# Two token tiles of the first MLP that are computed alone: the tile of 384 tokens is put ahead of the tile of 512

## The chip, the cores and the metric

The kernel runs on one core of one Trainium2 chip. The metric is the device time of one execution in microseconds (us), the median over several executions. PE is TensorE (PEld its weight loads), DVE is VectorE, ACT is ScalarE, POOL is GpSimd, SP is the engine whose queue issues most DMAs.

## The reference

Three stages follow one another, all in float32: attention over channels, a gated MLP and a second MLP.

```python
# q, k, v: (1, 6016, 256)
qn = q / (norm(q, axis=1) + 1e-6);  kn = k / (norm(k, axis=1) + 1e-6)
a = softmax(kn^T @ qn / tau)               # 256 x 256
x = v @ a                                  # 6016 x 256
g = x @ w_gate;  x = (silu(g) * (x @ w_val)) @ w_out       # d_ff = 1536
h = x @ w_in;    out = (h * clip(h + 3, 0, 6) / 6) @ w_out2  # d_ff = 2048
```

## The kernel before

The attention matrix is folded into the weights of the first MLP, so the first MLP reads v directly. Float32 products are made of parts: each operand is split into a high part (a rounded copy, fp32r) and a low part (what is left), and one product is three passes on PE: high x high, low x high, high x low (`PASSES`). A 128 x 128 block of weights is loaded for each pass.

The 6016 tokens are 11 tiles of 512 (`BANK`) and one of 384 (`REST`). Ten tiles of 512 go in five pairs, in which seven products stand for eight; the remaining two tiles go alone and first. Before the change tile 0 has 512 tokens and tile 1 has 384. The order of each engine's work is written out by hand, and semaphores tie the engines together:

- PE, `first_alone(i)` (tile i, 12 blocks j of 128 hidden channels, c = 12 i + j): `up(i, j)` is 12 matmuls (gate, then value), which may start when `prod_full` says that DVE has multiplied block c - 2, since the hidden values have two pairs of PSUM banks. From j = 3 on, `down` of block j - 3 follows each `up`: 6 matmuls, of which the first four wait for the high part (`prod_high`) and the last two for the low part (`prod_ready`) of that block. In tile 0 the last two blocks are done by `finish` (12 matmuls, one half of the output after the other, so that the first half already needs the low part of block 11). In tile 1 the last four `down`s are moved into the first two frames of the pairs. All matmuls of a tile are as wide as it has tokens.
- ACT: silu of the gate (L900); then in tile 0 the high part of tile 1's v (L904, behind blocks 5 and 6); in tile 1 casts of the first pair's operands.
- DVE, per block: the multiplication (L1243, one input in PSUM), the cast that makes the high part (L1233, SBUF to SBUF), the subtraction that makes the low part (L1151, two SBUF inputs). In tile 0 it also transposes tile 1's v (L1203, 2 instructions, behind blocks 4 and 5) and makes its low part (L1151 on `vT_odd`, behind blocks 7 and 8). In tile 1 it transposes v of the first pair (behind blocks 1 and 3).
- POOL meanwhile builds the weights of the pairs from the folded ones: `join_up` (L668, 12 instructions), `sum_up` (L675 four subtractions or additions, L689 four casts, L692 four subtractions, for each of three groups of blocks). Its group n = 1 stops ahead of the casts until tile 0's products are all split (`prod_ready`), then it goes on; later it prepares the first pair's operands (L707, L713).
- SP: loads v tile by tile into one buffer (`v_in`) and stores the two lone results (`y_alone`, L535).

These lines set the widths and what PE waits for:

```python
V_LAST_TURNED, V_LAST_CAST = (4, 5), (5, 6)
...
pe.wait_ge(prod_full, c - 1)
...
if n == 1:
    pool.wait_ge(prod_ready, 2 + J1)
```

Of the kernel before, what the change touches and what calls it, by code (L numbers as in the profile page):

```python
# [21 lines left out]
BANK = 512  # L22
# [4 lines left out]
def attention_mlp_mlp_kernel(nc, q, k, v, tau, w_gate, w_val, w_out, w_in2, w_out2, out):  # L27
# [8 lines left out]
    KC = C // P  # L36
    J1, J2 = F1 // P, F2 // P
    PAIRS = N // (2 * BANK)

    REST = N - (2 * PAIRS + 1) * BANK  # L40
# [15 lines left out]


    def tokens_at(n):
        return n * BANK if n < 2 else REST + (n - 1) * BANK

    def tokens_of(n):
        return REST if n == 1 else BANK


    def tile_of(pair, side):
        if pair < PAIRS:
            return 2 + 2 * pair + side
        return 2 + 2 * (pair - PAIRS - (pair > NARROWER)) + side
# [50 lines left out]
    with ctx:  # L119
        def sb(name, shape, dt=fp32, stack=ctx):  # L120
            return stack.enter_context(nc.sbuf_tensor(name, shape, dt))

        def sem(name):
            return ctx.enter_context(nc.semaphore(name))
# [17 lines left out]
        with ExitStack() as attention:  # L142
# [8 lines left out]
            vT_even = sb("vT_even", [P, 2, KC, BANK], fp32r, attention)  # L151
# [5 lines left out]
            with ExitStack() as early:  # L157
                vT_odd_raw = sb("vT_odd_raw", [P, 2, KC, BANK], fp32, early)
            vT_odd = sb("vT_odd", [P, 2, KC, BANK], fp32r, attention)
# [10 lines left out]
        with ExitStack() as first:  # L170
            up_w = sb("up_w", [P, J1, 7, 2, P], fp32r, first)
            down_w = sb("down_w", [P, J1, 2, C], fp32r, first)
# [23 lines left out]
        psum = ctx.enter_context(nc.psum_tensor("psum", [P, 8, BANK], fp32))  # L196
        HID = [psum[:, b, :] for b in range(4)]
        SUMS_OUT = [psum[:, 4 + b, :] for b in range(4)]
# [18 lines left out]
        NOTHING, ANYTHING = nc.const_aps.tensor(0.0, [P, P], fp32), nc.const_aps.tensor(1.0, [P, BANK], fp32)  # L217
        FOLD = [psum[:, 4 + r, :] for r in range(4)]
        SQ = [psum[:, 4 + 2 * h:6 + 2 * h, :].rearrange("p b c -> p (b c)") for h in range(2)]
        V_FIRST = [psum[:, c, :] for c in range(KC)]  # L220

        first_loaded = sem("first_loaded")
        first_squared = sem("first_squared")
# [44 lines left out]
        vT_high = sem("vT_high")  # L268
        vT_ready = sem("vT_ready")
# [45 lines left out]
        full = {x: sem(f"full_{x}") for x in ("L", "R", "1L", "2R", "2L", "1R")}  # L315
# [36 lines left out]
        def by_blocks(bank):  # L352
            return bank.rearrange("p (j c) -> p j c", c=P)
# [50 lines left out]
        V_TURNED = (4, 5)  # L404
# [59 lines left out]
        def pieces_of(pair, side):  # L464
            half, full, rest = (n // SQUARE for n in (HALF, BANK, REST))
            if pair != NARROWER:
                return ((tile_of(pair, side), 0, 0, full),)
            return ((0, half, 0, full - half), (1, 0, full - half, rest)) if side else ((0, 0, 0, half),)


        def stores_before(pair):
# [333 lines left out]
        def _(act):  # L805
# [52 lines left out]

            def vT_evict(c):
                act.wait_ge(v_read, c + 1)  # L860
                nc.scalar.copy(vT_even[:, 0, c, :], V_FIRST[c]).then_inc(vT_high, 1)

            def exponent(h):
                act.wait_ge(max_ready, h + 1)
# [13 lines left out]
            for r, (h, i) in enumerate(GROUPS_OF_FOLD):  # L878
                if r == TURNED_AT:
                    expT_evict(1)  # L880
                g, n = UP_BLOCKS[i]
# [9 lines left out]
            def cast_x(pair, k):  # L891
                act.wait_ge(x_summed, 4 * pair + {3: 2, 4: 3, 5: 4}.get(k, 1))
                nc.scalar.copy(XS[pair % 2][:, k, 0, 0:pair_width(pair)], raw_x(pair, k)).then_inc(x_high, 1)  # L893

            def first_alone(i):
                for j in range(J1):
                    c = i * J1 + j
                    act.wait_ge(gate_ready, c + 1)
                    act.wait_ge(prod_ready, c + 1)
                    nc.scalar.activation(act_out[:, j % 2, 0:tokens_of(i)], HID[2 * j % 4][:, 0:tokens_of(i)], ACT.Silu).then_inc(act_ready, 1)  # L900
                    if i == 0 and j in V_LAST_CAST:
                        b = V_LAST_CAST.index(j)
                        act.wait_ge(v_read, KC + b + 1)
                        nc.scalar.copy(vT_odd[:, 0, b, 0:REST], vT_odd_raw[:, 1, b, 0:REST]).then_inc(vT_high, 1)  # L904
                    if i == 1 and j >= J1 - 7:
                        cast_x(0, j - (J1 - 7))
                if i == 0:
                    keep_y_alone(i)

            def keep_y_alone(i):  # L910
                for c in range(KC):
                    act.wait_ge(y_summed, KC * i + c + 1)
                    if i > 0:
                        act.wait_ge(y_alone_stored, 32)
                    nc.scalar.copy(y_alone[:, c, 0:tokens_of(i)], SUMS_OUT[2 * i + c][:, 0:tokens_of(i)]).then_inc(y_alone_kept, 1)
# [165 lines left out]
        def _(dve):  # L1081
# [31 lines left out]
            half = 2 * C  # L1113
# [36 lines left out]
            def low(dst, full, high):  # L1150
                return nc.vector.tensor_tensor(dst, full, high.bitcast(fp32), ALU.subtract)  # L1151
# [48 lines left out]
            def turn_v(n, c, turned, tokens=BANK):  # L1200
                if c == 0:
                    dve.wait_ge(v_loaded, (n + 1) * (16 * GROUPS))
                nc.vector.transpose(turned.rearrange("p (m t) -> p m t", t=SQUARE),  # L1203
                                    v_in[:, c:tokens // SQUARE * KC:KC, :]).then_inc(v_read, 1)

            def vT_evict(c):
                dve.wait_ge(vT_high, c + 1)
                low(vT_even[:, 1, c, :], V_FIRST[c], vT_even[:, 0, c, :]).then_inc(vT_ready, 1)

            for r, (h, i) in enumerate(GROUPS_OF_FOLD):  # L1210
                if r == TURNED_AT:
                    expT_low(1)
                g, n = UP_BLOCKS[i]
                high, lo = (folded_up(g, h, part, n) for part in range(2))
                dve.wait_ge(fold_high, r + 1)
                nc.vector.scalar_tensor_tensor(lo, by_blocks(FOLD[r % 4]), row_rec[:, h:h + 1], high.bitcast(fp32),
                                               ALU.mult, ALU.subtract).then_inc(fold_ready, 1)
                if r in V_TURNED:
                    turn_v(0, V_TURNED.index(r), V_FIRST[V_TURNED.index(r)])
                if r in TURNED:  # L1220
                    vT_evict(TURNED.index(r))

# [14 lines left out]
            def first_alone(i):  # L1237
                for j in range(J1):
                    c = i * J1 + j
                    a = act_out[:, j % 2, 0:tokens_of(i)]  # L1240
                    dve.wait_ge(act_ready, c + 1)
                    dve.wait_ge(val_ready, c + 1)
                    nc.vector.tensor_tensor(a, HID[(2 * j + 1) % 4][:, 0:tokens_of(i)], a, ALU.mult).then_inc(prod_full, 1)  # L1243
                    split(c)
                    if i == 0 and j in V_LAST_TURNED:
                        b = V_LAST_TURNED.index(j)
                        turn_v(1, b, vT_odd_raw[:, 1, b, 0:REST], REST)
                    if i == 0 and j - 2 in V_LAST_CAST:
                        b = V_LAST_CAST.index(j - 2)
                        dve.wait_ge(vT_high, KC + b + 1)  # L1250
                        low(vT_odd[:, 1, b, 0:REST], vT_odd_raw[:, 1, b, 0:REST],
                            vT_odd[:, 0, b, 0:REST]).then_inc(vT_ready, 1)
                    if i == 1 and j in (1, 3):
                        turn_x(0, j // 2)

# [120 lines left out]
            for i in range(2):  # L1376
                b = LAST_BLOCKS - 2 + i
# [4 lines left out]
        def _(pe):  # L1382
# [105 lines left out]
            for r, (h, i) in enumerate(GROUPS_OF_FOLD):  # L1488
                if r == TURNED_AT:
                    turn_exp(1)  # L1490
                g, n = UP_BLOCKS[i]
# [29 lines left out]
            def down(c, n, banks, w, j, last=False):  # L1521
                pe.wait_ge(prod_high, c + 1)
                for part, m in PASSES:
                    if m == 1:
                        pe.wait_ge(prod_ready, c + 3)
                    for h in range(KC):
                        end = mm(banks[h][:, 0:n], w[:, j, part, h * P:(h + 1) * P], prod[:, c % 4, m, 0:n],  # L1527
                                 start=j == 0 and (part, m) == PASSES[0], stop=last and (part, m) == PASSES[-1])
                        if last and (part, m) == PASSES[-1]:
                            end.then_inc(y_summed, 1)  # L1530
                if not last:
                    end.then_inc(prod_used, 1)
# [89 lines left out]
            def downs_of(f, half):  # L1622
                if f < 2:

                    j = J1 - 4 + 2 * f + half
                    down(J1 + j, REST, SUMS_OUT[2:4], down_w, j, last=j == J1 - 1)
                elif f < SECOND:
                    down_first(f - 2, half)
                elif f == SECOND:
                    for side in range(2):  # L1630
                        down_first(SECOND - 2 + half, side)
                else:
                    for x in ORDER2[2 * half:2 * half + 2]:
                        if (f, x) != (FRAMES - 1, ORDER2[-1]):
                            down_second(f - 1, x)
# [90 lines left out]
```

## Time and profile before

| | before |
|---|---|
| median of 3 runs | 1086.69 us (1086.4 to 1087.62) |
| the profiled execution's own time | 1086.27 us |
| its span, first to last instruction | 1084.5 us |
| PE busy | 1080.3 us |
| DVE, ACT, POOL busy | 780.2, 667.3, 327.7 us |
| tile 0 on PE | 61.18 to 110.14 us |
| tile 1 on PE, up to the first frame | 110.14 to 143.45 us |

A row of the timeline gives the start and the length of an instruction or of a merged run of them, its engine and line, the operation, the tile it writes and those it reads, the shapes, and the count; in brackets stands the idle time before it and what ended it. Matmuls overlap: the step from one start to the next is what one costs, the length also holds its way through the array.

### The profile page before, as it was taken

What the parts mean: (1) busy time and instruction counts of PE and PEld (TensorE: products, weight loads), DVE (VectorE), ACT (ScalarE), POOL (GpSimd) and SP (SyncE); (2) the same over time, 40 slices, a digit from 0 to 9 for tenths busy, and PEclk for the clock granted to TensorE, in tenths of its full rate; (3) what the DMA queues carried; (4) which work ended last, traced back from release to release, by engine and by line L of the source; (5) the groups of instructions that cost most, each with busy time, mean ns of one, the idle gap of its engine ahead of it and who ended that gap; (6) DMA issues with size and microseconds to landing.
All of it is one profiled execution on the core that took longest, in us unless ns stands there. A gap on an engine that the chain in (4) does not pass through costs nothing.

```text
span 1084.5 us, 14748 instructions
## 1 busy us (share of the span) xinstructions
PE 1080.3 (100%) x5052; PEld 915.3 (84%) x5052; DVE 780.2 (72%) x1146; ACT 667.3 (62%) x1169; POOL 327.7 (30%) x247
## 2 busy tenths in 40 slices
PE   9999999999999999999999999999999999999998
PEld 7888998888888888888888888998888888888998
DVE  6788779666666766766678776776776776776766
ACT  8731245665665565566577776676666666666655
POOL 7998545200310220223088431220210210210000
PEclk9999999999999999999999999999999999999999
DMA  9711112002102100101122201111011111110111
GB/s 381 249 34 20 40 34 40 1 1 59 20 1 59 21 1 20 40 1 39 59 59 72 79 1 32 25 24 40 18 18 39 20 20 40 20 20 1 21 20 40
DMA packets 111082, 46.83 MB, mean 43 GB/s; under 512 B 91552, under 2 KB 101024, under 8 KB 111008
## 3 DMA queue, kind: packets, MB, share of 16 engines
q1 hardware_dynamic: 110432, 44.71, 15.0%
q10 hardware_dynamic: 576, 1.18, 0.3%
q8 instruction: 41, 0.67, 0.3%
q14 instruction: 33, 0.27, 0.1%
HBM read 33.55 MB, written 12.32 MB: 42 GB/s over the span
## 4 chain that ended last, share of the span: by engine, by line
PE 99%; DMA 0%; DVE 0%; DVEq 0%; issue 0%
PE psum L1573 47%; PE psum L1595 35%; PE psum L1517 5%; PE psum L1582 4%; PE psum L1527 2%; PE psum L1395 2%; PE psum L1499 2%; PE psum L1427 1%; PE psum L1408 0%; DMA qk_first<-in_k 0%; PE psum L1541 0%; PE psum L1461 0%; PE psum L1474 0%; PE psum L1483 0%; DVE out_sb L1379 0%; PE psum L1693 0%
## 5 line engine op out<-in xcount | busy, mean ns | idle before, releaser
L1595 PE MATMUL psum<-prod,down_w 128*128 128x512 f32 (+1 forms) x1680 | 408.4, 386 | 0.0
L1595 PEld LDWEIGHTS psum<-prod,down_w 128*128 128x128 f32 x1680 | 315.3, 188 | 61.1 <-DVE y_right L1293 0.2
L1573 PE MATMUL psum<-x_even,up_w 128*128 128x512 f32 (+1 forms) x1260 | 302.8, 386 | 0.0
L1573 PEld LDWEIGHTS psum<-x_even,up_w 128*128 128x128 f32 x1260 | 235.4, 188 | 44.5 <-ACT slots L945 0.3
L1573 PE MATMUL psum<-x_odd,up_w 128*128 128x512 f32 x1008 | 245.3, 389 | 0.0
L1573 PEld LDWEIGHTS psum<-x_odd,up_w 128*128 128x128 f32 x1008 | 189.1, 188 | 39.6 <-DVE more_slots L1318 0.4
L1273 DVE TENSOR_TENSOR slots<-psum,slots 128x512 f32<-128x512 f32 (+1 forms) x108 | 74.1, 686 | 122.9 <-ACT slots L953 96.6
L1322 DVE SCALAR_TENSOR_TENSOR prod<-slots,prod 128x512 fp32r<-128x512 f32 (+1 forms) x144 | 100.7, 700 | 32.8 <-ACT prod L996 28.3
L1318 DVE SCALAR_TENSOR_TENSOR slots<-slots 128x512 f32<-128x512 f32 (+1 forms) x120 | 84.2, 701 | 38.0 <-ACT slots L1006 38.0
L996 ACT ACTIVATE prod<-slots 128x512 fp32r<-128x512 f32 (+1 forms) x144 | 90.0, 625 | 28.2 <-DVE slots L1318 28.2
L713 POOL TENSOR_TENSOR x_even<-x_even_raw,x_even 128x512 fp32r<-128x512 f32 (+1 forms) x42 | 54.0, 1295 | 159.5 <-ACT x_even L893 159.5
L1006 ACT ACTIVATE slots<-slots 128x512 f32<-128x512 f32 (+1 forms) x120 | 75.1, 626 | 34.7 <-DVE slots L1273 31.4
L1151 DVE TENSOR_TENSOR prod<-slots,prod 128x512 fp32r<-128x512 f32 x120 | 95.7, 798 | 0.0
L921 ACT CAST prod<-slots 128x512 fp32r<-128x512 f32 x120 | 74.6, 622 | 19.6 <-DVE slots L1278 11.7
L707 POOL TENSOR_TENSOR x_even_raw<-x_even_raw 128x512 f32<-128x512 f32 (+1 forms) x24 | 34.5, 1451 | 167.6 <-DVE x_even_raw L1203 90.2
L1269 DVE TENSOR_TENSOR slots<-psum,slots 128x512 f32<-128x512 f32 (+1 forms) x108 | 73.6, 682 | 8.5 <-PE psum L1573 8.5
L1264 DVE TENSOR_TENSOR slots<-psum,slots 128x512 f32<-128x512 f32 (+1 forms) x84 | 57.3, 682 | 30.4 <-PE psum L1573 30.1
L713 POOL TENSOR_TENSOR x_odd<-x_odd_raw,x_odd 128x512 fp32r<-128x512 f32 x28 | 35.9, 1292 | 121.2 <-ACT x_odd L893 121.2
L707 POOL TENSOR_TENSOR x_odd_raw<-x_odd_raw 128x512 f32<-128x512 f32 x20 | 29.4, 1481 | 122.2 <-PE psum L1573 66.6
L959 ACT ACTIVATE slots<-slots 128x512 f32<-128x512 f32 x60 | 38.1, 635 | 43.5 <-DVE slots L1273 43.5
L937 ACT COPY slots<-psum 128x512 f32<-128x512 f32 x60 | 35.3, 589 | 40.0 <-PE psum L1573 40.0
L1006 ACT ACTIVATE more_slots<-psum 128x512 f32<-128x512 f32 (+1 forms) x48 | 28.3, 589 | 50.7 <-PE psum L1573 50.5
(151 smaller groups left out, 1309.6 us busy)
## 6 DMA issues: line engine op xcount, KB each, us to landing
out<-out_sb SPq DMA_DIRECT2D x38, 128.0 KB, 2.6
v_in<-in_v SPq DMA_DIRECT2D x36, 128.0 KB, 3.2
qk<-in_q SPq DMA_DIRECT2D x8, 512.0 KB, 9.2
qk<-in_k SPq DMA_DIRECT2D x7, 512.0 KB, 10.5
x_odd_raw<-y_rows SPq DMA_DIRECT2D x12, 256.0 KB, 3.3
y_rows<-act_out SPq DMA_DIRECT2D x10, 256.0 KB, 2.1
y_rows<-y_right SPq DMA_DIRECT2D x10, 256.0 KB, 3.0
down_raw<-in_moe_w_out SPq DMA_DIRECT2D x4, 512.0 KB, 3.8
```

Source lines behind the costliest of these rows:

```text
L707: nc.gpsimd.tensor_tensor(raw_x(pair, k), raw_x(pair, a), raw_x(pair, b), ALU.subtract).then_inc(x_summed, 1)
L713: nc.gpsimd.tensor_tensor(low, raw_x(pair, k), high.bitcast(fp32), ALU.subtract).then_inc(x_ready, 1)
L921: nc.scalar.copy(buffer_of(f, x)[:, 0, :], gated_left if x == "L" else kept6(f)).then_inc(high_of[x], 1)
L996: nc.scalar.activation(buffer_of(f, x)[:, 0, :], clipped(x, f), ACT.Copy, scale=1.0 / 6.0).then_inc(high_of[x], 1)
L1006: nc.scalar.activation(clipped(x, f), src, ACT.Relu, bias=3.0).then_inc(relu_of[x], 1)
L1151: return nc.vector.tensor_tensor(dst, full, high.bitcast(fp32), ALU.subtract)
L1269: nc.vector.tensor_tensor(kept1(f), left_sums(f), kept1(f), ALU.add).then_inc(row1_left, 1)
L1273: nc.vector.tensor_tensor(kept7(f), right_sums(f), kept7(f), ALU.add).then_inc(row2_right, 1)
L1318: nc.vector.scalar_tensor_tensor(clipped(x, f), clipped(x, f), 6.0, hidden, ALU.min, ALU.mult).then_inc(full[x], 1)
L1322: nc.vector.scalar_tensor_tensor(buffer_of(f, x)[:, 1, :], clipped(x, f), 1.0 / 6.0, buffer_of(f, x)[:, 0, :].bitcast(fp32), ALU.mult, ALU ...
L1573: end = mm(bank, w[:, u, k, part, :], XS[pair % 2][:, k, m, 0:pair_width(pair)], start=start and (part, m) == PASSES[0], stop=stop and (pa ...
L1595: end = mm(sums_out(pair_of(f), side, h), w[:, j, part, h * P:(h + 1) * P], buffer_of(f, x)[:, m, :], start=start and (part, m) == PASSES[ ...
```

## The change

`tokens_of` gives 384 to tile 0 and 512 to tile 1, and `tokens_at` shifts with it; the views of tile 0 are narrowed and those of tile 1 widened. Each engine issues the same instructions in the same order. The number of matmuls at each width stays the same.

```diff
     def tokens_at(n):
-        return n * BANK if n < 2 else REST + (n - 1) * BANK
+        return 0 if n == 0 else REST + (n - 1) * BANK
 
     def tokens_of(n):
-        return REST if n == 1 else BANK
+        return REST if n == 0 else BANK
...
-        V_FIRST = [psum[:, c, :] for c in range(KC)]
+        V_FIRST = [psum[:, c, 0:REST] for c in range(KC)]
...
             if pair != NARROWER:
                 return ((tile_of(pair, side), 0, 0, full),)
-            return ((0, half, 0, full - half), (1, 0, full - half, rest)) if side else ((0, 0, 0, half),)
+            return ((1, half - rest, 0, half),) if side else ((0, 0, 0, rest), (1, 0, rest, half - rest))
...
-                        nc.scalar.copy(vT_odd[:, 0, b, 0:REST], vT_odd_raw[:, 1, b, 0:REST]).then_inc(vT_high, 1)
+                        nc.scalar.copy(vT_odd[:, 0, b, :], vT_odd_raw[:, 1, b, :]).then_inc(vT_high, 1)
...
-                        turn_v(1, b, vT_odd_raw[:, 1, b, 0:REST], REST)
+                        turn_v(1, b, vT_odd_raw[:, 1, b, :])
...
-                        low(vT_odd[:, 1, b, 0:REST], vT_odd_raw[:, 1, b, 0:REST],
-                            vT_odd[:, 0, b, 0:REST]).then_inc(vT_ready, 1)
+                        low(vT_odd[:, 1, b, :], vT_odd_raw[:, 1, b, :],
+                            vT_odd[:, 0, b, :]).then_inc(vT_ready, 1)
...
-                    down(J1 + j, REST, SUMS_OUT[2:4], down_w, j, last=j == J1 - 1)
+                    down(J1 + j, BANK, SUMS_OUT[2:4], down_w, j, last=j == J1 - 1)
```

On DVE, from the second transposition of tile 1's v in tile 0 to the second subtraction for tile 1's v, the kernel before has these instructions (L1243, L1233, L1151 on `prod` are one block's multiplication, cast and low part):

```order
 L1203 STREAM_TRANSPOSE vT_odd_raw<-v_in 128x384
 L1243 TENSOR_TENSOR act_out<-psum,act_out 128x512
 L1233 CAST prod<-act_out 128x512
 L1151 TENSOR_TENSOR prod<-act_out,prod 128x512
 L1243 TENSOR_TENSOR act_out<-psum,act_out 128x512
 L1233 CAST prod<-act_out 128x512
 L1151 TENSOR_TENSOR prod<-act_out,prod 128x512
 L1151 TENSOR_TENSOR vT_odd<-vT_odd_raw,vT_odd 128x384
```

The changed kernel has in that place:

```order
 L1203 STREAM_TRANSPOSE vT_odd_raw<-v_in 128x512
 L1243 TENSOR_TENSOR act_out<-psum,act_out 128x384
 L1233 CAST prod<-act_out 128x384
 L1151 TENSOR_TENSOR prod<-act_out,prod 128x384
 L1243 TENSOR_TENSOR act_out<-psum,act_out 128x384
 L1233 CAST prod<-act_out 128x384
 L1151 TENSOR_TENSOR prod<-act_out,prod 128x384
 L1151 TENSOR_TENSOR vT_odd<-vT_odd_raw,vT_odd 128x512
```

The instructions and their order are the same; those of tile 0 became narrower and those for tile 1's v wider. POOL's list is the same in both kernels. On SP the loads of v and the two stores of `y_alone` change their sizes, each in its place:

```order
-L501 DMA v_in<-in_v 32x32x32 x4
+L501 DMA v_in<-in_v 32x24x32 x4
 L523 DMA w_stage<-in_moe_w_out 128x4x256 x3
-L501 DMA v_in<-in_v 32x24x32 x4
+L501 DMA v_in<-in_v 32x32x32 x8
+L535 DMA y_rows<-y_alone 128x384 x2
 L501 DMA v_in<-in_v 32x32x32 x4
 L535 DMA y_rows<-y_alone 128x512 x2
-L501 DMA v_in<-in_v 32x32x32 x4
-L535 DMA y_rows<-y_alone 128x384 x2
```

No transfer was moved past another.

## Rows read from the trace of the kernel before

**Rows 1.** The page: span, busy time of each engine, PE over 40 slices.

```profile
span 1084.5 us, 14748 instructions
PE 1080.3 (100%) x5052; PEld 915.3 (84%) x5052; DVE 780.2 (72%) x1146; ACT 667.3 (62%) x1169; POOL 327.7 (30%) x247
PE   9999999999999999999999999999999999999998
```

**Rows 2.** Windows of tile 0 and tile 1: busy us of each engine, clock, DMA.

```profile
61.18:110.14 48.96, 48.96 (x217) 40.55 (x216) 39.69 (x42) 9.49 (x16) 44.54 (x34) 1.00 0.08 13
110.14:143.45 33.31, 33.31 (x193) 33.30 (x192) 26.12 (x37) 10.00 (x20) 18.24 (x14) 1.00 0.14 32
```

**Rows 3.** Timeline of PE, first blocks of tile 0, its end, tile 1.

```profile
61.18 0.39 PE L1517 MATMUL psum<-vT_even,gate_w 128*128 128x512 f32 x1
...
63.90 0.39 PE L1517 MATMUL psum<-vT_even,gate_w 128*128 128x512 f32 x1
...
107.42 2.88 PE L1541 MATMUL psum<-prod,down_w 128*128 128x512 f32 x12
110.14 0.33 PE L1517 MATMUL psum<-vT_odd,gate_w 128*128 128x384 f32 x1
...
112.25 0.33 PE L1517 MATMUL psum<-vT_odd,gate_w 128*128 128x384 f32 x1
...
114.33 0.33 PE L1517 MATMUL psum<-vT_odd,gate_w 128*128 128x384 f32 x1
```

**Rows 4.** Timeline of DVE in tile 0, first block, block 3, start of block 4.

```profile
64.17 0.69 DVE L1243 TENSOR_TENSOR act_out<-psum,act_out 128x512 f32<-128x512 f32 x1 [1.25 <-PE psum L1517]
...
73.98 0.68 DVE L1243 TENSOR_TENSOR act_out<-psum,act_out 128x512 f32<-128x512 f32 x1
74.69 0.81 DVE L1233 CAST prod<-act_out 128x512 fp32r<-128x512 f32 x1
75.54 1.66 DVE L1151 TENSOR_TENSOR prod<-act_out,prod 128x512 fp32r<-128x512 f32 x1
77.13 0.68 DVE L1243 TENSOR_TENSOR act_out<-psum,act_out 128x512 f32<-128x512 f32 x1
```

**Rows 5.** Timeline of POOL during tile 0.

```profile
87.46 2.83 POOL L689 CAST up_w<-up_raw 128x512 fp32r<-128x512 f32 x4
90.26 6.47 POOL L692 TENSOR_TENSOR up_w<-up_raw,up_w 128x512 fp32r<-128x512 f32 x4
96.69 6.10 POOL L675 TENSOR_TENSOR up_raw<-up_raw 128x512 f32<-128x512 f32 x4
106.99 2.29 POOL L689 CAST up_w<-up_raw 128x512 fp32r<-128x512 f32 x4 [4.19 <-DVE prod L1151]
```

**Rows 6.** Timeline of DVE in tile 1, one block beside POOL and the next.

```profile
128.13 0.55 DVE L1243 TENSOR_TENSOR act_out<-psum,act_out 128x384 f32<-128x384 f32 x1
128.71 0.87 DVE L1233 CAST prod<-act_out 128x384 fp32r<-128x384 f32 x1
129.61 1.53 DVE L1151 TENSOR_TENSOR prod<-act_out,prod 128x384 fp32r<-128x384 f32 x1
131.07 0.55 DVE L1243 TENSOR_TENSOR act_out<-psum,act_out 128x384 f32<-128x384 f32 x1
```

**Rows 7.** Timeline of DVE in tile 0: work for tile 1's v, and after.

```profile
80.26 0.57 DVE L1203 STREAM_TRANSPOSE vT_odd_raw<-v_in 128x384 f32<-128x384 f32 x1
80.76 0.65 DVE L1243 TENSOR_TENSOR act_out<-psum,act_out 128x512 f32<-128x512 f32 x1
81.44 0.43 DVE L1233 CAST prod<-act_out 128x512 fp32r<-128x512 f32 x1
...
95.50 1.64 DVE L1151 TENSOR_TENSOR vT_odd<-vT_odd_raw,vT_odd 128x384 fp32r<-128x384 f32 x1
...
106.16 0.69 DVE L1151 TENSOR_TENSOR prod<-act_out,prod 128x512 fp32r<-128x512 f32 x1
```

**Rows 8.** Timeline of DVE in tile 1 with POOL idle, and a late load.

```profile
115.58 0.36 DVE L1233 CAST prod<-act_out 128x384 fp32r<-128x384 f32 x1
115.98 0.56 DVE L1151 TENSOR_TENSOR prod<-act_out,prod 128x384 fp32r<-128x384 f32 x1
116.45 1.30 DVE L1203 STREAM_TRANSPOSE x_even_raw<-v_in 128x512 f32<-128x512 f32 x2
...
123.74 1.31 DVE L1203 STREAM_TRANSPOSE x_even_raw<-v_in 128x512 f32<-128x512 f32 x2 [3.10 <-DMA v_in<-in_v]
```

More of the change, by code:

```diff
@@ L860, in vT_evict @@
                 act.wait_ge(v_read, c + 1)
-                nc.scalar.copy(vT_even[:, 0, c, :], V_FIRST[c]).then_inc(vT_high, 1)
+                nc.scalar.copy(vT_even[:, 0, c, 0:REST], V_FIRST[c]).then_inc(vT_high, 1)
             def exponent(h):
@@ L1207, in vT_evict @@
                 dve.wait_ge(vT_high, c + 1)
-                low(vT_even[:, 1, c, :], V_FIRST[c], vT_even[:, 0, c, :]).then_inc(vT_ready, 1)
+                low(vT_even[:, 1, c, 0:REST], V_FIRST[c], vT_even[:, 0, c, 0:REST]).then_inc(vT_ready, 1)
             for r, (h, i) in enumerate(GROUPS_OF_FOLD):
@@ L1218, in _ @@
                 if r in V_TURNED:
-                    turn_v(0, V_TURNED.index(r), V_FIRST[V_TURNED.index(r)])
+                    turn_v(0, V_TURNED.index(r), V_FIRST[V_TURNED.index(r)], REST)
                 if r in TURNED:
```

## The prediction, as put on record before the changed kernel ran

> **What bounds the kernel now.** I read the page first: PE is busy for 1080.3 of 1084.5 us and at 9 in all slices but the last [rows 1]. The chain that ended last is PE for 99% of the span, so nothing on another engine costs time unless it opens a gap in PE's stream, and a change that leaves PE's work alone can win next to nothing. The windows of the two lone tiles come next: PE is busy for 48.96 of 48.96 us in tile 0 and 33.31 of 33.31 us in tile 1, at a granted clock of 1.00 [rows 2]. But in tile 0 POOL is busy for 44.54 and DVE for 39.69 us as well; this is where the three meet. The timelines then say how close DVE is to PE there.
>
> **PE's own work.** A 512-wide matmul costs (63.90 - 61.18) / 12 = 0.2267 us, a 384-wide one (114.33 - 112.25) / 12 = 0.1733 us [rows 3]. Each tile has 216 of them (144 up, 72 down), before and after. Both sums merely swap places: 216 x 0.2267 = 48.96, which is tile 0's window, becomes 216 x 0.1733 = 37.43 us. Without a gap, tile 1 would start at 61.18 + 37.43 = 98.62 instead of 110.14, and tile 1 with its four late downs would end as far behind that as to cancel it. So the pure count gives no change.
>
> **DVE's pace.** In tile 0 a block takes DVE 77.13 - 73.98 = 3.15 us [rows 4], while PE needs 18 x 0.2267 = 4.08 us for an up and a down. DVE has 0.93 us to spare per block, and pays out of that for tile 1's v. A block is that long because of POOL: the cast is 0.81 and the low part 1.66 us [rows 4]; with POOL idle and 384 wide they are 0.36 and 0.56 [rows 8]. The pattern is one of turns: either of the two instructions waits for a POOL instruction to end, and one POOL instruction gets in behind each. So a block costs about two POOL instructions, whose length (1.27 us from start to start when alone, as I take it from the steps within this pattern) does not depend on the tile. The nearest row at the new width is in tile 1, where POOL works on other 512-wide tiles: 131.07 - 128.13 = 2.94 us per block at 384 [rows 6]. That is only 0.21 less than at 512. PE's block, however, falls from 4.08 to 18 x 0.1733 = 3.12 us. The spare time falls from 0.93 to 0.18 us a block, and tile 1's v, now 512 wide, has to be paid from it.
>
> The page "SBUF — State Buffer" of the Trainium skill, section "Who interferes with whom", says that a DVE instruction with two SBUF inputs, or in a two-port mode, and a GpSimd instruction that reads SBUF exclude each other for the whole instruction. By full exclusion a block would be 0.36 + 0.56 plus two POOL instructions of 1.30, an estimate of 3.52 us; the row's 2.94 lies below it, and the row decides.
>
> **DVE's sum in tile 0.** Block 0's multiplication starts 0.27 us behind the end of its up (64.17 against 63.90, [rows 3, 4]); now 61.18 + 2.08 + 0.27 = 63.53. Its low part ends about 2.82 us later, at 66.35. The low parts of blocks 1 to 4 follow at 2.94 us each: 78.11. PE allows that: up of block 4 starts at 70.54, and block 2 is multiplied by 69.9.
>
> Blocks 5 and 6 have a transposition ahead, 512 wide: 0.69 us instead of 0.57 (two take 1.30 to 1.31 less their overlap [rows 8]). It needs no turn, so it lies beside a POOL instruction. Before, transposition and multiplication together just filled that instruction, and the cast came at 81.44 and took its bare 0.43 us [rows 7]. Now 0.12 more and 0.10 to 0.13 less (0.55 against 0.65 to 0.68) leave the cast within 0.03 us of where it was, at the edge: if it gets in, the block costs 3.07 us, if it just misses, POOL goes first and the block costs 1.14 us more, 4.21 us. Both values go into the sum as cases.
>
> From block 7 to 9 there are two more subtractions for v, each a further turn: 1.64 us by the row at 384 [rows 7], 1.7 at 512. Against that stands that POOL's four casts take 2.83 us in all, 0.71 each [rows 5], not 1.45: DVE's turns are shorter for some 3 us. Turn by turn, behind block 4 at 78.11: with the casts in, blocks 5 and 6 at 3.07 each give 84.25; block 7 at 2.94, 87.19; block 8 with the first v subtraction would be 2.94 + 1.6, less 1.4 for two to three turns at a POOL cast, so 3.15, 90.34; block 9 with the second is 2.94 + 1.70 = 4.64, 94.98; blocks 10 and 11 at 2.94, **100.86**. If the casts miss, blocks 5 and 6 at 4.21 give 86.53, but then the POOL casts fall together with blocks 7 and 8 (2.14 and 3.95), and POOL's list (28 instructions from 63.27 on) runs out before the last block, which takes 1.96: **102.16**. The same walk for the kernel before gives 106.85 for its last low part, and the row is 106.16 + 0.69 = 106.85 [rows 7]; there DVE waits for PE, so this proves the pace less than the turns.
>
> **What PE feels.** Until block 9 it hardly stalls. Up of block 11 needs block 9's multiplication, which ends near 92.5 to 95, against 92.38 on a full schedule: up to 2 us. `finish` needs the low part of block 11 for its sixth matmul; behind that one stand 6 more, and with 0.1 us for the semaphore, tile 1 starts 7 x 0.1733 + 0.1 = 1.31 us behind that low part: 102.17 or 103.47. Against 98.62 this is **3.55 or 4.85 us** late. Before, `finish` started at 107.42 [rows 3] and its sixth matmul came at 108.55, 1.7 us behind the low part.
>
> Nothing gives this back. Tile 1 is 512 wide, PE needs 4.08 us per block from block 3 on, DVE 3.15; POOL's second group starts at once when the last low part is done, as before [rows 5]. The load of v that DVE waits for 3.10 us in tile 1 [rows 8] had almost no room before; now it has about 3 us, since the blocks around it are longer for PE. The four late downs stay covered by casts made long before. Stores, the wider eviction of `y_alone` (0.11 us each) and the split of the stores of the narrower pair lie beside full PE: nothing. The narrower v of tile 0 is ready ahead of the fold's end: nothing.
>
> **Sum.** The profiled execution: 1084.5 + 4.2 (between the two cases, which I hold about equal) = 1088.7 us of span, 1090.5 us of time. Its own time, 1086.27, is 0.42 below the median of the runs, so the forecast is 1086.69 + 4.2 = **1090.9 us**. If POOL's 1.27 is 1.24 or 1.30 the loss moves by 0.65 us either way, so the forecast case reaches from 2.9 to 5.6 us: 1089.6 to 1092.3.
>
> **Rivals.**
> 1. *DVE keeps up, no change.* It speaks for it that 2.94 is below 3.12, and that POOL may run out of work before tile 0 ends. Against it: after the two v subtractions there are no spare microseconds to catch up, and POOL's list lasts until 102.8 now [rows 5]. It decides at the last low part: with no loss it must end by 98.62 - 1.31 = 97.3, and below 99.5 the loss is under 2.2 us. Time 1086.7, up to 1088.9. 0.13.
> 2. *PE's clock or the frames behind suffer too.* The gaps in PE's stream, near 1.5 us before block 11 and about 3 us in pieces within `finish`, are the first in this stretch; all windows before read 1.00. Were the clock halved after them for one up of tile 1, that alone is 2.7 us: 1093.6, and more if it lasts. Against it: the gaps have matmuls between them. 0.06.
> 3. *Faster: narrow matmuls run closer to their columns.* In tile 1 weight loads are busy for 33.30 of 33.31 us [rows 2], so the 0.1733 us is perhaps the loads' pace, not the 384 columns / 2.4 GHz = 0.160 us. If tile 0 gave it at 0.160, 216 x 0.0133 = 2.9 us would be won, 1083.8, provided DVE followed. It decides at 0.163 us per matmul, and nothing about the new place speaks for it. 0.02. The page "TensorE: Matmul & The Clock Gate" of the Trainium skill, section "Back-to-back issue gap", gives N / 2.4 + 2.5 ns, so 0.1625 us here; the rows contradict it for both widths.
>
> The forecast has the other 0.79. A measurement of this kernel tells about 0.2% (2.2 us) from no change. Slower: 0.79 + 0.06 = 0.85; within: 0.13; faster: 0.02. The range leaves out the lower part of rival 1 and the upper part of rival 2: 1088.6 to 1093.0.
>
> **What would show it.** In the changed kernel's timeline DVE should run without waiting for PE from block 1 to block 11 of tile 0, at 2.9 to 3.0 us per block; the casts after the two transpositions should read 0.36 (in) or about 1.5 us (missed). The last low part should end at 100 to 103 us, up of block 11 and `finish` should have gaps before or in them, and tile 1 should start at 102 to 103.5. From there to the end every piece should be as long as before. I am wrong if tile 1 starts before 100.5, if DVE's block at 384 beside L668 and L675 is clearly under 2.8 us, or if a second loss shows in the first frames.

## The result and the profile after

| | before | changed |
|---|---|---|
| median | 1087.38 us (6 runs) | 1091.6 us (6 runs, 1089.3 to 1092.33) |
| ratio, 95% interval | | 1.0037 [1.0024, 1.005] |
| profiled execution, its own time | 1086.27 us | 1089.3 us |
| its span | 1084.5 us | 1087.5 us |

The changed kernel is slower by 4.2 us. The profiled execution shows only 3.0 of them; it is the fastest of the six and the only one whose mean granted clock was 1.000 (the others 0.997 to 0.998). So there are two parts to find.

The page of the changed kernel, against [rows 1]:

```profile
span 1087.5 us, 14748 instructions
PE 1080.5 (99%) x5052; PEld 915.2 (84%) x5052; DVE 779.5 (72%) x1146; ACT 667.3 (61%) x1169; POOL 327.2 (30%) x247
```

The busy times are those of before to 0.7 us: no engine has more to do, and 2.8 of the 3.0 us are idle time of PE (1087.5 - 1080.5 = 7.0 against 4.2). The waits of PE say who held it (us in total, times, longest):

```profile
PE psum L1541 <- DVE prod L1151: 1.5, 2, 0.9
PE psum L1541 <- DVE prod L1233: 0.9, 1, 0.9
```

L1541 is `finish` of tile 0. The timeline of DVE there, the answer to [rows 4, 7]: block 4 beside POOL, the first transposition with what follows it, the two subtractions for tile 1's v, the start of block 9, block 11, and the first multiplication of tile 1.

```profile
75.26 0.54 DVE L1243 TENSOR_TENSOR act_out<-psum,act_out 128x384 f32<-128x384 f32 x1
75.84 0.87 DVE L1233 CAST prod<-act_out 128x384 fp32r<-128x384 f32 x1
76.74 1.53 DVE L1151 TENSOR_TENSOR prod<-act_out,prod 128x384 fp32r<-128x384 f32 x1
78.20 0.70 DVE L1203 STREAM_TRANSPOSE vT_odd_raw<-v_in 128x512 f32<-128x512 f32 x1
78.83 0.51 DVE L1243 TENSOR_TENSOR act_out<-psum,act_out 128x384 f32<-128x384 f32 x1
79.38 0.36 DVE L1233 CAST prod<-act_out 128x384 fp32r<-128x384 f32 x1
...
87.16 1.09 DVE L1151 TENSOR_TENSOR vT_odd<-vT_odd_raw,vT_odd 128x512 fp32r<-128x512 f32 x1
...
90.31 1.77 DVE L1151 TENSOR_TENSOR vT_odd<-vT_odd_raw,vT_odd 128x512 fp32r<-128x512 f32 x1
92.00 0.54 DVE L1243 TENSOR_TENSOR act_out<-psum,act_out 128x384 f32<-128x384 f32 x1
...
97.85 0.54 DVE L1243 TENSOR_TENSOR act_out<-psum,act_out 128x384 f32<-128x384 f32 x1
98.43 0.84 DVE L1233 CAST prod<-act_out 128x384 fp32r<-128x384 f32 x1
99.31 1.51 DVE L1151 TENSOR_TENSOR prod<-act_out,prod 128x384 fp32r<-128x384 f32 x1
105.23 0.69 DVE L1243 TENSOR_TENSOR act_out<-psum,act_out 128x512 f32<-128x512 f32 x1 [4.41 <-PE psum L1517]
```

The cast and the low part at 384 read 0.87 and 1.53, as in [rows 6]; the cast behind the transposition takes its bare 0.36. No row between 63.71 and 105.23 has a wait in brackets: DVE is the bound of tile 0. Its last low part ends at 99.31 + 1.51 = 100.82. POOL beside blocks 10 and 11:

```profile
96.11 5.84 POOL L675 TENSOR_TENSOR up_raw<-up_raw 128x512 f32<-128x512 f32 x4
```

These four take 1.46 us each, and DVE's block 2.93 us: two POOL instructions to a block. And PE at that place, after [rows 3]:

```profile
94.81 2.24 PE L1527 MATMUL psum<-prod,down_w 128*128 128x384 f32 x12
96.89 0.51 PE L1541 MATMUL psum<-prod,down_w 128*128 128x384 f32 x2
97.98 0.45 PE L1541 MATMUL psum<-prod,down_w 128*128 128x384 f32 x1 [0.58 <-DVE prod L1151]
99.33 0.62 PE L1541 MATMUL psum<-prod,down_w 128*128 128x384 f32 x2 [0.90 <-DVE prod L1233]
100.87 1.49 PE L1541 MATMUL psum<-prod,down_w 128*128 128x384 f32 x7 [0.93 <-DVE prod L1151]
```

Three gaps, for block 10's low part, block 11's high part and block 11's low part. A bracket counts from the end of the row before it. Counted from when the next matmul was due, 0.173 us behind the start of the last one, PE lost 0.74, 1.18 and 1.19 us. Tile 1's first matmuls come at 102.2; at full pace they would have come at 61.33 (the start of tile 0 here) + 37.44 = 98.77. That is 3.4 us late, 3.1 of it in the three gaps.

### The profile page after: what moved, and what is told of

Its sections match the earlier page's. It is cut to its first block, busy times and chain, and to the rows that moved or that the text cites. A ratio compares the mean times of both kernels' runs of the same rounds, so it can differ in the third digit from the quotient of the medians.

```text
span 1087.5 us, 14748 instructions
## 1 busy us (share of the span) xinstructions
PE 1080.5 (99%) x5052; PEld 915.2 (84%) x5052; DVE 779.5 (72%) x1146; ACT 667.3 (61%) x1169; POOL 327.2 (30%) x247
## 3 DMA queue, kind: packets, MB, share of 16 engines
q10 hardware_dynamic: 576, 1.18, 0.3%
## 4 chain that ended last, share of the span: by engine, by line
PE 98%; DVE 1%; DMA 0%; issue 0%; DVEq 0%
PE psum L1573 47%; PE psum L1595 35%; PE psum L1517 5%; PE psum L1582 4%; PE psum L1395 2%; PE psum L1527 2%; PE psum L1499 2%; PE psum L1427 1%; PE psum L1408 0%; DMA qk_first<-in_k 0%; DVE prod L1233 0%; DVE vT_odd L1151 0%; DVE prod L1151 0%; DVE act_out L1243 0%; PE psum L1541 0%
## 5 line engine op out<-in xcount | busy, mean ns | idle before, releaser
L1151 DVE TENSOR_TENSOR prod<-slots,prod 128x512 fp32r<-128x512 f32 x120 | 95.5, 796 | 0.0
```

## The experiments

The runs of one group share the executions of the kernel before. Its median is 1087.02 us (24 runs) beside the changed kernel again, the gaps filled, POOL held back before its second group's additions, and both tiles at 448 tokens. It is 1086.58 us (15 runs) beside the other four.

### The changed kernel again

Nothing is edited.

> The changed kernel once more. In its profiled execution tile 0 ends in three gaps of PE (0.58, 0.90 and 0.93 us) and the granted clock was 1.000, with a time of 1089.3 us; five unprofiled executions read 1091.2 to 1092.3 us at a clock of 0.997 to 0.998. Theory A (two terms): the gaps cost about 3 us always, and in most executions the gaps also bring the clock down for a stretch, 2 to 3 us more. It expects times in two groups, near 1089.3 at 1.000 and near 1091.7 at 0.998, and if the profile falls in the second group, a stretch of lower clock at or soon behind the gaps, some 2 to 3 us of added length there. Theory B (one term, the spread is noise of the whole run): times spread evenly between 1089 and 1092.5 with no tie to the clock, and the kernel before spreads as widely.

Measured: 1091.41 us (1091.09 to 1092.26, 5 runs), ratio 1.0043 [1.003, 1.0055]. All five have a clock of 0.997 or 0.998; all 24 of the kernel before have 1.000 and spread from 1086.25 to 1088.39. With the runs above that is ten executions at 0.997 or 0.998 between 1091.1 and 1092.3 us, and one at 1.000 with 1089.3. This time the profile caught the lower clock. PE's timeline, from the third gap on:

```profile
101.09 2.22 PE L1541 MATMUL psum<-prod,down_w 128*128 128x384 f32 x7 [0.93 <-DVE prod L1151]
103.10 0.63 PE L1517 MATMUL psum<-vT_odd,gate_w 128*128 128x512 f32 x1
103.53 0.63 PE L1517 MATMUL psum<-vT_odd,up_w 128*128 128x512 f32 x1
...
104.38 0.63 PE L1517 MATMUL psum<-vT_odd,up_w 128*128 128x512 f32 x1
104.81 0.47 PE L1517 MATMUL psum<-vT_odd,gate_w 128*128 128x512 f32 x1
```

The seven matmuls take 2.22 instead of 1.49 us, and the next ones step by 0.43 us instead of 0.227: 1.2 GHz instead of 2.4, until about 104.8. The windows of this execution (columns as in [rows 2]) say the same by the granted clock:

```profile
98.00:102.50 4.50, 2.48 (x9) 1.90 (x10) 2.96 (x4) 0.48 (x1) 4.36 (x4) 0.90 0.00 0
102.50:106.00 3.50, 3.50 (x12) 2.95 (x11) 0.00 (x0) 0.92 (x2) 3.50 (x6) 0.65 0.30 112
106.00:110.00 4.00, 4.00 (x19) 3.27 (x19) 2.92 (x3) 0.75 (x2) 3.70 (x3) 1.00 0.00 0
```

In the execution with the clock at 1.000 the same three windows all read 1.00, though the gaps are as long there; why that one kept its clock is open. The first frame starts at 147.56 here and at 145.76 there; 0.2 us of the difference was there before the gaps (101.09 against 100.87), so the clock costs 1.6 us. Theory A holds as to the two groups; its 2 to 3 us were too much.

### The gaps filled

13 matmuls whose result nobody reads stand in the three gaps.

```diff
+                def idle(count):
+                    for _ in range(count):
+                        mm(SUMS_OUT[3][:, 0:n], up_of(0, 0, 0, 0), vT[0][:, 0, 0, 0:n], start=True, stop=True)
+
+                pe.wait_ge(fold_ready, len(GROUPS_OF_FOLD))
                 order = [(k, h, p) for h in range(KC) for k in range(2) for p in PASSES]
                 for i, (k, h, (part, m)) in enumerate(order):
+                    idle({2: 3, 3: 5, 5: 5}.get(i, 0))
```

> The changed kernel with 13 extra matmuls of 384 columns (0.173 us each, 2.25 us in all) that write a bank nobody reads, placed 3, 5 and 5 in the three gaps of the finish of tile 0. Theory A (gaps lower the clock): tile 1 starts at 102.2 us as before to 0.2 us, the clock reads 1.000 in all executions, and all times are near 1089.3: 2.2 us less than the changed kernel. Theory B (the clock or the spread has nothing to do with the gaps): the times stay at the changed kernel's, median 1091.6, or rise a little.

Measured: 1089.7 us (1089.35 to 1090.14, 8 runs), ratio 1.0025 [1.0014, 1.0035], clock 1.000 in all eight. The kernel issues more and is 1.7 to 1.9 us faster than the changed one. Its timeline of PE shows the gaps nearly closed and the rest in place (tile 1 starts at 102.25):

```profile
97.24 0.68 PE L1537 MATMUL psum<-vT_even,gate_w 128*128 128x384 f32 x3
97.98 0.44 PE L1547 MATMUL psum<-prod,down_w 128*128 128x384 f32 x1
98.27 1.03 PE L1537 MATMUL psum<-vT_even,gate_w 128*128 128x384 f32 x5
99.35 0.62 PE L1547 MATMUL psum<-prod,down_w 128*128 128x384 f32 x2
```

That separates the two parts: 1089.7 - 1087.0 = 2.7 us are the stall, the remaining 1.7 to 1.9 us the clock, and the clock falls because of the gaps. Which of the three gaps it takes for that, the run does not say.

### POOL held back before its second group's additions

```diff
                 pool.wait_ge(up_joined, 4 * n + 4)
+                if n == 1:
+                    pool.wait_ge(prod_ready, 2 + J1)
                 summed(1, row2_first, row2_second, ALU.add)
```

> The changed kernel, but POOL waits for the end of tile 0's products ahead of the four L675 additions of its second group, not only behind them. Theory A (DVE is slow in tile 0 because it takes turns with POOL): from about 96.1 us on DVE's block 10 and 11 take their bare 1.5 us, the last low part ends near 98.5 instead of 100.8, tile 1 starts near 99.8 instead of 102.2, and the time falls by about 2.4 us in executions at the same clock: 1086.9 with the clock at 1.000. Rival (DVE's pace comes from its own chain with ACT and PE): the last low part stays at 100.8 and the time with it.

Measured: 1087.09 us (1086.77 to 1087.69, 11 runs), ratio 0.9999 [0.9991, 1.0008], clock 1.000. Blocks 10 and 11 on DVE, with POOL idle from 96.9 on, and POOL's four additions when it has them to itself:

```profile
96.22 0.86 DVE L1235 CAST prod<-act_out 128x384 fp32r<-128x384 f32 x1
97.12 0.56 DVE L1153 TENSOR_TENSOR prod<-act_out,prod 128x384 fp32r<-128x384 f32 x1
97.59 0.55 DVE L1245 TENSOR_TENSOR act_out<-psum,act_out 128x384 f32<-128x384 f32 x1
98.18 0.36 DVE L1235 CAST prod<-act_out 128x384 fp32r<-128x384 f32 x1
98.57 0.56 DVE L1153 TENSOR_TENSOR prod<-act_out,prod 128x384 fp32r<-128x384 f32 x1
99.28 5.17 POOL L675 TENSOR_TENSOR up_raw<-up_raw 128x512 f32<-128x512 f32 x4 [2.41 <-DVE prod L1153]
```

Block 11 starts 1.95 us behind block 10, and its three instructions run bare. POOL gains as well: 1.29 us an addition instead of 1.46. The last low part ends at 99.13. This execution began tile 0 0.47 us later than the profiled one above (block 0's multiplication at 64.18 against 63.71), so in like terms it ends at 98.66, 2.2 us earlier, as expected. One gap of 0.29 us is left in PE, and tile 1, at 100.53, is still 1.3 us behind the full pace (61.81 + 37.44 = 99.25). POOL did the same work later, and no engine waited for it. Deferring four instructions takes away the whole loss that the times can show: their interval allows 0.9 us.

### The two subtractions for tile 1's v left out

The low part of tile 1's v is filled with zeros instead of being computed.

```diff
-                        low(vT_odd[:, 1, b, :], vT_odd_raw[:, 1, b, :],
-                            vT_odd[:, 0, b, :]).then_inc(vT_ready, 1)
+                        nc.vector.memset(vT_odd[:, 1, b, :].bitcast(fp32), 0.0).then_inc(vT_ready, 1)
```

> The changed kernel, but the two 512-wide subtractions that make the low part of tile 1's v are left out, and a fill with zeros stands in their place (that part of the computation is missing). Theory A (DVE's load in tile 0 is 12 blocks beside POOL plus the work for tile 1's v): the two took 1.09 + 1.77 us less overlap, a fill takes 0.3 to 0.6 us, so the last low part ends near 98.9 instead of 100.8 and tile 1 starts near 100.2 instead of 102.2; the time at clock 1.000 is near 1087.7. Rival (the pace of the blocks alone makes the lateness): the last low part stays beyond 100.3 us.

Measured: 1087.45 us (1087.13 to 1087.96, 10 runs), ratio 1.0003 [0.9994, 1.0013]. The clock is 1.000 in nine executions and 0.999 in the profiled one. The last low part ends at 97.30 + 1.51 = 98.81, tile 1 starts at 100.20:

```profile
97.30 1.51 DVE L1151 TENSOR_TENSOR prod<-act_out,prod 128x384 fp32r<-128x384 f32 x1
98.86 1.50 PE L1540 MATMUL psum<-prod,down_w 128*128 128x384 f32 x7 [0.93 <-DVE prod L1151]
```

Both as expected to 0.1 us. The pace of the blocks alone, 2.94 against PE's 3.12 us, leaves 1.4 us of the 3.4 (100.20 against 61.36 + 37.44 = 98.80), with the transpositions and the two fills (0.48 us each) still in it; the two subtractions make the other 2.0. Of the three gaps only the last is left, with its 0.93 us, and alone it hardly touches the clock. The time came out near the expectation, but it cannot tell 1087.45 from no change.

### POOL held back for all of tile 0

```diff
             pool.wait_ge(fold_ready, len(GROUPS_OF_FOLD))
+            pool.wait_ge(prod_ready, 2 + J1)
             for n in range(UPS):
```

> The changed kernel, but POOL does none of its list until tile 0's products are split. Theory A: DVE takes its bare times in tile 0 (0.55, 0.36 and 0.56 us, under 1.6 us a block), waits for PE, and tile 1 starts at 61.3 + 37.4 = 98.7 to 98.9 us with no gap of PE before it. The price comes later, since POOL's 39 us of work then end near 140 us and the first pair's operands (another 16 us) near 156: the first frames should wait for x_even, 10 us or more, so a time of 1097 to 1105 us. If DVE's pace were its own, the blocks would stay near 2.9 us.

Measured, one run: 1103.89 us, clock 0.992. DVE in tile 0, block 10, and the place where PE pays for it, with what ACT waited for:

```profile
91.63 0.56 DVE L1244 TENSOR_TENSOR act_out<-psum,act_out 128x384 f32<-128x384 f32 x1 [1.57 <-PE psum L1518]
92.23 0.36 DVE L1234 CAST prod<-act_out 128x384 fp32r<-128x384 f32 x1
92.62 0.56 DVE L1152 TENSOR_TENSOR prod<-act_out,prod 128x384 fp32r<-128x384 f32 x1
```

```profile
142.91 0.80 PE L1518 MATMUL psum<-vT_odd,gate_w 128*128 128x512 f32 x1 [15.51 <-DVE act_out L1244]
141.02 0.62 ACT L894 CAST x_even<-x_even_raw 128x512 fp32r<-128x512 f32 x1 [23.85 <-POOL x_even_raw L707]
```

A block takes DVE 1.5 us and then it waits 1.57 us for PE; tile 1's first matmuls come at 98.65 without a gap. With POOL away tile 0 has no stall, though the work for tile 1's v is all there: DVE is late only beside POOL. One expectation was wrong in its place: not the frames waited but tile 1 itself, for 15.5 us, since ACT's casts of the first pair's operands stand in its queue ahead of the later silus of tile 1 and wait for POOL. Behind this gap the granted clock reads 0.50 from 142.9 to 147.0 us.

### Both tiles at 448 tokens

```diff
     def tokens_at(n):
-        return 0 if n == 0 else REST + (n - 1) * BANK
+        return n * HALF if n < 2 else REST + (n - 1) * BANK
 
     def tokens_of(n):
-        return REST if n == 0 else BANK
+        return HALF if n < 2 else BANK
```

The views that had `REST` or all columns take `HALF` as well, and each side of the narrower pair is stored in one piece.

> Both lone tiles have 448 tokens. PE's pure count is the same, 432 matmuls at 0.200 us. Theory A (tile 0 stalls where DVE's work beside POOL, which hardly falls with the width, outlasts PE's, which does): PE's tile 0 is 43.2 us, to 104.5; DVE's blocks are near 3.04 us beside POOL and its last low part ends near 102.6, while it is needed by 103.0; so no gap, clock 1.000, and the time of the kernel before, 1087.0 to 1087.4. Rival (half the change gives half of the loss): 1089.3.

Measured: 1087.48 us (1087.09 to 1088.26, 11 runs), ratio 1.0006 [0.9997, 1.0015]. DVE's block 9 to 10 beside POOL, and `finish`:

```profile
94.46 0.61 DVE L1243 TENSOR_TENSOR act_out<-psum,act_out 128x448 f32<-128x448 f32 x1
...
97.50 0.61 DVE L1243 TENSOR_TENSOR act_out<-psum,act_out 128x448 f32<-128x448 f32 x1
...
102.05 1.60 DVE L1151 TENSOR_TENSOR prod<-act_out,prod 128x448 fp32r<-128x448 f32 x1
```

```profile
102.84 2.60 PE L1541 MATMUL psum<-prod,down_w 128*128 128x448 f32 x12
```

A block takes 97.50 - 94.46 = 3.04 us, between 2.94 and 3.15, as expected. The last low part ends at 103.65, 1 us later than I said; the sixth matmul of `finish` is due at 102.84 + 5 x 0.203 = 103.85. PE runs through with 0.2 us to spare. The time is 0.1 us above the expected range; the interval ends at 1.6 us above the kernel before and so excludes the rival's 2.3. So the loss does not go with the width in proportion: it sets in where DVE's sum outlasts PE's, and half of the change costs nothing that can be measured.

### One gap in the kernel before: two sizes

The widths are those of before. DVE gets additions of 512 columns, each waiting for the last, ahead of the last low part of tile 0: five in the first kernel (shown), eight in the second.

```diff
                 dve.wait_ge(prod_high, c + 1)
+                if c == J1 - 1:
+                    for k in range(5):
+                        step(nc.vector.tensor_tensor(y_right[:, 0, :], full_sum, full_sum, ALU.add))
                 low(lo, full_sum, high).then_inc(prod_ready, 1)
```

> The kernel before (tile 0 512 wide), with five DVE additions of 512 columns, each waiting for the last, put between the cast and the low part of tile 0's last block, so near 0.75 us each. PE's sixth matmul of the finish then comes at 110.7 instead of 108.55: one gap of about 2.1 us, with PE full on both sides. If any gap of this sum lowers the clock, the time rises by 2.1 + 1.7 = 3.8 us, to 1090.8, at a clock of 0.998. If it takes the broken-up 4 us of the changed kernel (2.4 us idle in 4 us, with few matmuls between), the clock stays at 1.000 and the time is 1089.1.

Measured: 1090.06 us (1089.89 to 1090.66, 6 runs), ratio 1.0032 [1.002, 1.0044]. Clock 0.998 in five executions, 1.000 in the profiled one (1089.89). The waits of PE in it:

```profile
PE psum L1544 <- DVE prod L1151: 1.8, 1, 1.8
PE psum L1520 <- DVE act_out L1246: 1.1, 1, 1.1
```

This run is inconclusive as to the clock. There is a second gap that I had not foreseen: at 384 columns tile 1 has little room for DVE's wait for v, which was 4.07 us here against 3.10 in [rows 8], and PE stands for 1.1 us. The two gaps, 2.9 us, are about what the profiled execution lost (3.3 us), yet the executions at 0.998 are only 0.1 to 0.8 us longer than it. Where the lower clock lay in them no profile shows.

> As the run before, but with eight additions: one gap of about 4.4 us. Theory A (an idle stretch lowers PE's clock, and the stretch at 1.2 GHz then costs 1.7 us or more): clock 0.998 in all executions, time 1087.0 + 4.4 + 1.7 = 1093.1. Rival (the clock fell in the changed kernel for another reason than idle time): clock 1.000, time 1091.4.

Measured: 1093.47 us (1093.09 to 1093.89, 4 runs), ratio 1.0061 [1.0046, 1.0076], clock 0.997 in all four. PE at the gap and behind it, and the windows:

```profile
113.30 3.35 PE L1544 MATMUL psum<-prod,down_w 128*128 128x512 f32 x7 [4.00 <-DVE prod L1151]
116.45 0.52 PE L1520 MATMUL psum<-vT_odd,gate_w 128*128 128x384 f32 x1
```

```profile
108.00:112.00 4.00, 1.29 (x6) 0.75 (x4) 3.80 (x7) 0.00 (x0) 0.00 (x0) 0.93 0.00 0
112.00:116.00 4.00, 2.70 (x6) 2.15 (x7) 1.21 (x2) 0.59 (x1) 2.62 (x5) 0.50 0.11 41
116.00:120.00 4.00, 4.00 (x18) 3.88 (x17) 0.34 (x1) 1.08 (x2) 4.00 (x4) 0.71 0.23 90
```

The gap is 4.0 us, and PE has no wait behind it in tile 1 this time. The clock falls within it and stays at 0.50 until after 116 us. The seven matmuls behind the gap take 116.45 - 113.30 = 3.15 us instead of 7 x 0.2267 = 1.59, and the next ones step by 0.32 instead of 0.173 us until 118. The time is 6.9 us above before: 4.0 for the gap and 2.9 for the rest. The clock makes about 2.4 of that (1.56, then 0.73 and 0.14 in the up that follows); `finish` also began 0.6 us later in this execution, at 108.00 against 107.42. This is what theory A said, to 0.4 us: one gap, if it is long enough, lowers the clock in a kernel with the old widths too.

## Why the prediction came out right, and what in it was off

**PE's own count** was right: busy times did not move, and tile 1 at full pace would have started at 98.62 plus the 0.15 us by which this execution began tile 0 later.

**DVE's pace beside POOL** was right: 2.93 to 2.94 us per block, as in tile 1's rows, from which I took it. The three runs with POOL held back, in part or for all of the tile, and with the v work left out show the mechanism (DVE is slow beside POOL and at its bare pace without it) and its two parts.

**The turns one by one** gave 100.86 for the last low part with the casts in; it ended at 100.82, though the tile began 0.15 to 0.18 us later. Both casts after the transpositions got in (0.36 us), in every profile of a kernel with these widths. I had held the two cases to be equal and took the middle, 4.2 us; the right term was 3.55. The upper end of the forecast case should have been 4.85 + 0.65 = 5.5 us, not 5.6.

**What PE feels** was right as to `finish`. Tile 1 started 102.20 - 98.77 = 3.4 us late. Of the gap before block 11, for which I allowed up to 2 us, only 0.1 to 0.2 us came: block 9's multiplication ended at 92.00 + 0.54 = 92.54, where the up was due at 92.53.

**"Nothing gives this back"** was wrong by a small amount. Tile 1 began 3.4 us late, and tile 0 itself 0.15 us later than before: 3.6 us in all. Frame 2 starts at 155.97 before and 159.36 after, frame 5 at 178.79 and 181.85: 3.6 us becomes 3.39 and then 3.06. Up to frame 5 the kernel before lost 0.5 us in stretched matmuls, which the changed one did not; no run shows why. So the stall costs 3.0 us in the profiled executions and 2.7 by the medians with the gaps filled.

**The clock** was the step that failed, and with it "from there to the end every piece should be as long as before". I gave it 0.06 as a rival and a price of 2.7 us; it came in ten of eleven executions and costs 1.6 us by the two profiles, 1.7 to 1.9 by the medians. That is less than the 2.7, since behind the seven matmuls of `finish` only four or five of tile 1's ran at the lower clock. "The gaps have matmuls between them" was the argument against, and it does not hold: one matmul between the first and the second gap and two between the second and the third did not prevent it.

So the forecast of 4.2 us met the measured 4.2 us by two errors of opposite sign: the stall was taken 1.2 to 1.5 us too large, and the clock was left out. The direction and its cause stand by experiment; the agreement of the number is in part luck.

Of the other rivals, that DVE keeps up is what even tiles and POOL held back for all of tile 0 brought about, and nearly so POOL held back in part and the v work left out (1.3 and 1.4 us late); as a forecast for the change it was wrong. Faster matmuls in tile 0 did not come: the up rows step by 0.173 us there as well. The formula that rival 3 takes from the page "TensorE: Matmul & The Clock Gate" of the Trainium skill, section "Back-to-back issue gap", is given there for an isolated matmul, so these streams of weight loads and matmuls are no test of it.

## What to carry to other kernels

When a tile is made narrower, ask of each engine which of its costs shrink. PE's fell with the columns from 4.08 to 3.12 us a block, while DVE's, set by turns with POOL's 512-wide instructions, fell only from 3.15 to 2.94: a stage with 23% to spare became one with 6%, less than its side work needs. The cure is to move the neighbour's work that is not due yet (four POOL instructions here), not to make the instructions that wait shorter.

Expect a gap in PE's stream to cost more than its length once gaps come close together or one is long: three of 0.58 to 0.93 us with one and two matmuls between them did here in ten executions of eleven, and one of 4.0 us in four of four, while a single one of 0.93 us did not. And look at the granted clock of every execution, not of the profiled one alone: here the profile was the one execution in six without the second cost.

## What the runs showed of the hardware

- After three gaps of 0.58, 0.90 and 0.93 us, with three 384-column matmuls between them, PE went from 2.4 to 1.2 GHz, from within the seven matmuls that start at 101.09 us until about 104.8 us, in the execution that shows it; the mean clock, 0.997 or 0.998 in ten executions of eleven, fits that. PE had been busy for 36.56 of the 37.00 us from 61.00 to 98.00, most of the rest being the start of the first gap.
- The same place with 13 extra matmuls in the gaps kept 1.000 in eight of eight. One gap of 0.93 us (the two subtractions left out) left it at 1.000 in nine executions and 0.999 in one; one gap of 4.00 us lowered it in four of four.
- A DVE block of three instructions costs about two 512-wide POOL instructions (1.46 us each there, 1.29 alone) beside POOL, nearly whatever its width: 2.94 us at 384, 3.04 at 448, 3.15 at 512, against 1.5 bare at 384. A transposition of 0.70 us added to it costs 0.1 (79.77 - 76.74 = 3.03 us from one low part to the next).
